# Three small weight computations of an attention stage: from VectorE to GpSimd

## The reference

```python
B, H, S, D = 4, 8, 576, 64
a = softmax(causal(q @ k.T / sqrt(D)));  local = a @ v
q_p = phi(q)                      # phi(x) = x + 1 for x > 0, else exp(x)
mem_out = (q_p @ M_prev) / (q_p @ z_prev + 1e-6)
g = sigmoid(beta)                 # one gate for each head
attn = g * mem_out + (1 - g) * local
# then x = attn as (2304, 512); two layers up/down, 512 -> 2048 -> 512,
# the first with a clipped square as activation, the second with silu
```

## Time and profile before

| | us |
|---|---|
| median of 3 runs | 987.01 (986.19 to 989.4) |
| the profiled execution | 988.2 |
| its span in the trace | 986.1 |
| attention stage: until TensorE's first feed-forward matmul | 193.6 |

### The profile page before, as it was taken

One profiled execution on the slowest core, in us unless ns is written; L12 is line 12 of the kernel. 1 busy time (PEld: TensorE's weight loads), 2 busy tenths in 40 slices (PEclk: granted clock), 3 DMA queues, 4 the chain that ended last, 5 costly groups with the idle time before them and its releaser, 6 DMA issues.

```text
span 986.1 us, 14130 instructions
## 1 busy us (share of the span) xinstructions
PE 975.1 (99%) x5468; PEld 816.0 (83%) x5468; DVE 474.3 (48%) x946; ACT 384.1 (39%) x847; POOL 285.6 (29%) x304
## 2 busy tenths in 40 slices
PE   7999999999999999999999999999999999999998
PEld 6888877888888888888888998888888888888897
DVE  6999999756344434434434663323332332322232
ACT  6988888633223222322223332322222232222232
POOL 6989999799000000000000798000000000000000
PEclk8999999999999999999999999999999999999999
DMA  6555544244000000000000343001000100100010
GB/s 196 150 157 154 168 145 131 71 119 117 22 1 1 1 0 1 1 1 1 1 1 1 86 129 97 0 1 43 1 1 1 44 0 1 43 1 1 1 44 22
DMA packets 38401, 48.10 MB, mean 49 GB/s; under 512 B 3264, under 2 KB 21696, under 8 KB 38336
## 3 DMA queue, kind: packets, MB, share of 16 engines
q1 hardware_dynamic: 38336, 47.20, 15.9%
HBM read 42.47 MB, written 4.72 MB: 48 GB/s over the span
## 4 chain that ended last, share of the span: by engine, by line
PE 83%; DVE 8%; POOL 3%; issue 2%; ACT 2%; DMA 1%; SPq 0%; POOLq 0%; DVEq 0%
PE ps L1021 26%; PE ps L1023 26%; PE ps L1022 26%; PE ps L899 2%; PE ps L954 1%; DVE prob L653 1%; DVE qlo L635 1%; PE ps L862 1%; DVE ptail L653 1%; DVE mden L659 1%; DVE rw L685 1%; POOL phir L358 1%; ACT prob L476 1%; DVE glo L797 1%; POOL phs L386 1%
## 5 line engine op out<-in xcount | busy, mean ns | idle before, releaser
L1021 PE MATMUL ps<-xhi,W 128*128 128x512 f32 (+1 forms) x640 | 235.4, 368 | 0.0
L1022 PE MATMUL ps<-xlo,W 128*128 128x512 f32 (+1 forms) x640 | 235.4, 368 | 0.0
L1023 PE MATMUL ps<-xhi,W 128*128 128x512 f32 (+1 forms) x640 | 235.4, 368 | 0.0
L797 DVE TENSOR_TENSOR glo<-act_t,ghi 128x512 fp32r<-128x512 f32 (+1 forms) x160 | 118.0, 738 | 223.6 <-ACT ghi L576 223.6
L576 ACT CAST ghi<-act_t 128x512 fp32r<-128x512 f32 (+1 forms) x160 | 92.5, 578 | 235.4 <-PE ps L1023 213.1
L1021 PEld LDWEIGHTS ps<-xhi,W 128*128 128x128 f32 x640 | 120.7, 189 | 20.7
L1022 PEld LDWEIGHTS ps<-xlo,W 128*128 128x128 f32 x640 | 120.6, 188 | 20.4
L1023 PEld LDWEIGHTS ps<-xhi,W 128*128 128x128 f32 x640 | 120.6, 188 | 20.2
L335 POOL CAST W<-stage 128x512 fp32r<-128x512 f32 x64 | 46.2, 722 | 303.0 <-PE ps L1023 300.6
L568 ACT ACTIVATE act_t<-act_t,half_col 128x512 f32<-128x512 f32 (+1 forms) x80 | 54.5, 681 | 185.7 <-DVE act_t L790 185.7
L1021 PE MATMUL ps<-ghi,W 128*128 128x512 f32 (+1 forms) x320 | 118.1, 369 | 0.3 <-DVE glo L797 0.2
(11 more groups left out here) (113 smaller groups left out, 1336.5 us busy)
## 6 DMA issues: line engine op xcount, KB each, us to landing
stage<-in_moe_w_in SPq DMA_DIRECT2D x32, 256.0 KB, 2.7
stage<-in_moe_w_out SPq DMA_DIRECT2D x32, 256.0 KB, 2.7
vn<-in_vN SPq DMA_DIRECT2D x16, 320.0 KB, 5.0
qraw<-in_qT SPq DMA_DIRECT2D x15, 320.0 KB, 3.2
qn<-in_qN SPq DMA_DIRECT2D x16, 288.0 KB, 4.9
zb<-in_zN SPq DMA_DIRECT2D x32, 144.0 KB, 3.6
out_x<-ostage SPq DMA_DIRECT2D x17, 256.0 KB, 2.0
kraw<-in_kT SPq DMA_DIRECT2D x15, 288.0 KB, 2.9
```

Of the source, the lines that this page charges most:

```text
L797: nc.vector.tensor_tensor(glo[:, f % SLOTS, 0:TN[tile]], a, ghi[:, f % SLOTS, 0:TN[tile]].bitcast(F32), ALU.subtract).then_inc(glo_done, 1)
L1021: nc.tensor.matmul(dst, w_lo_, x_hi_, start=first, stop=False)
L1022: nc.tensor.matmul(dst, w_hi_, x_lo_, start=False, stop=False)
L1023: return nc.tensor.matmul(dst, w_hi_, x_hi_, start=False, stop=last)
```

## The change

GpSimd computes three things that VectorE computed: the gate's product (into a new tile `share`), phi's weights `rw[:, 1]`, and the last block's weights `rwt`. GpSimd does them between `phi_sum_1(p+1)` and `weigh(p)`, each waiting for the one before it. VectorE keeps the reduce, the addition of 1e-9 and the two reciprocals. In the first pair VectorE does `rows` ahead of `norms`.

```diff
+        share = sb("share", [P, NB], where=att)
+            def shares(p):
+                pool.wait_ge(norm_step, 2 * p + 2)
+                if p == 0:
+                    pool.wait_ge(gate_step, 5)
+                nc.gpsimd.tensor_tensor(share[:], mden[:, 1], gcols[:, p % PAIRS, :], ALU.mult).then_inc(gated, 1)
+
+            def weights(p):
+                pool.wait_ge(gated, p + 1)
+                pool.wait_ge(row_step, 2 * p + 1)
+                nc.gpsimd.tensor_tensor(rw[:, 1, :], den[:], share[:], ALU.mult).then_inc(row_made, 1)
+                pool.wait_ge(row_step, 2 * p + 2)
+                pool.wait_ge(row_made, 2 * p + 1)
+                nc.gpsimd.tensor_tensor(rwt[:], rw[:, :, 2 * FULL:].broadcast_to([P, 2, 2]),
+                                        bd[:].unsqueeze(1).broadcast_to([P, 2, 2]), ALU.mult).then_inc(row_made, 1)
+
             def weigh(p):
-                pool.wait_ge(row_step, 4 * p + 4)
+                pool.wait_ge(row_made, 2 * p + 2)
...
             for p in range(NPAIR):
                 if 0 < p < NPAIR - 1:
                     phi_sum_1(p + 1)
+                shares(p)
+                weights(p)
                 weigh(p)
                 widen(p)
...
-                elif step == 1:
-                    dve.wait_ge(norm_step, 3 * p + 1)
+                else:
+                    dve.wait_ge(norm_step, 2 * p + 1)
                     if p:
-                        dve.wait_ge(row_step, 4 * p - 1)
+                        dve.wait_ge(gated, p)
                     nc.vector.reciprocal(mden[:, 1], mden[:, 0]).then_inc(norm_step, 1)
-                else:
-                    dve.wait_ge(norm_step, 3 * p + 2)
-                    dve.wait_ge(gate_step, 5)
-                    nc.vector.tensor_tensor(mden[:, 1], mden[:, 1], gcols[:, p % PAIRS, :],
-                                            ALU.mult).then_inc(norm_step, 1)
...
                 if step == 0:
                     dve.wait_ge(exp_done, NB * p + NB)
+                    if p:
+                        dve.wait_ge(row_made, 2 * p)
                     nc.vector.tensor_scalar(den[:], rowsum[:, p % 2, :], 1e-9, None, ALU.add).then_inc(row_step, 1)
...
-                elif step == 2:
-                    dve.wait_ge(norm_step, 3 * p + 3)
-                    if p:
-                        dve.wait_ge(weighed, 2 * p)
-                    nc.vector.tensor_tensor(rw[:, 1, :], den[:], mden[:, 1], ALU.mult).then_inc(row_step, 1)
-                else:
-                    nc.vector.tensor_tensor(rwt[:], rw[:, :, 2 * FULL:].broadcast_to([P, 2, 2]),
-                                            bd[:].unsqueeze(1).broadcast_to([P, 2, 2]), ALU.mult).then_inc(row_step, 1)
...
                 if p == 0:
+                    for step in range(2):
+                        rows(0, step)
                     norms(0, 0)
                     norms(0, 1)
-                    norms(0, 2)
-                    for step in range(4):
-                        rows(0, step)
```

More of the change, by code:

```diff
@@ L189, in build @@
         norm_step, row_step, row_wide = sem("norm_step"), sem("row_step"), sem("row_wide")
+        gated, row_made = sem("gated"), sem("row_made")
         weighed, v_done = sem("weighed"), sem("v_done")
@@ L464, in phi_part_2 @@
                 if p >= 2:
-                    act.wait_ge(norm_step, 3 * p - 5)
+                    act.wait_ge(norm_step, 2 * p - 3)
                 nc.scalar.activation(phie[p % 2][:, :, 0:D], phir[p % 3][:], ACT.Exp, scale=-1.0).then_inc(phi_part, 1)
@@ L673, in rows @@
                     dve.wait_ge(exp_done, NB * p + NB)
+                    if p:
+                        dve.wait_ge(row_made, 2 * p)
                     nc.vector.tensor_scalar(den[:], rowsum[:, p % 2, :], 1e-9, None, ALU.add).then_inc(row_step, 1)
-                    return
-                dve.wait_ge(row_step, 4 * p + step)
-                if step == 1:
+                else:
+                    dve.wait_ge(row_step, 2 * p + 1)
                     if p:
@@ L775, in _ @@
                 if more:
-                    for step in range(3):
+                    for step in range(2):
                         norms(p + 1, step)
```

## The result

The changed kernel takes 989.12 us (median of 22 runs, 987.8 to 990.88), the one before 986.86 (22 runs, 985.93 to 989.4). The ratio is 1.0024, with a 95% interval of 1.0018 to 1.0030: slower by 2.3 us, inside the 0.3% that I took for no change, and clear of zero. Predicted were +0.8 us and the range 984.3 to 992.0.

The account below looks back on a forecast made before the run. Attention pairs were bound by TensorE and GpSimd; GpSimd's added chain, 15 x 0.80, less 11.3 us of former waits, gave +0.7, so 988.9 profiled and 987.8 us as median, range 984.3 to 992.0.

Parts of the forecast that it names:

- TensorE's floor: Attention stage: TensorE needs 11.05 us a pair without a split; the stage holds 3.1 + 0.5 = 3.6 us above that.
- GpSimd becomes the sole bound of pairs 5 to 14: Two pairs would take GpSimd 23.16 us, before 22.70, against 22.10 for TensorE.
- c: GpSimd's three added dependent operations, from the end of L353 to the start of L386: 0.80 us, bounded by 0.40 and 1.15.
- the line through L389 and L386: GpSimd tensor_tensor length from two rows: 1.67 ns an element and 0.19 fixed, hence 0.20 to 0.21 for small ones.
- 15c - 11.3: Shift of the kernel's end: 15 times c, minus GpSimd's former waits for VectorE; here +0.7 us.
- L386 of pairs 2, 8, 14 and 15: Forecast start times of GpSimd's `weigh` in these pairs: near 41.4, 109.1, 178.5 and 187.5 us.
- The wait of 2.54 in the last pair: GpSimd's former wait for VectorE in pair 15; it would absorb most of the delay, from +2.6 to +0.9 us.
- TensorE's scores are late by 0.65: GpSimd's `high_k(15)` in pair 13 comes 2.1 us later, VectorE wins back 1.47, so scores are 0.65 late.
- by way of L377: Last pair: L377, which TensorE's L933 needs, comes 0.9 us later, so L933 and all after it 0.7 later.
- VectorE wins 1.47 at a turn with a hold: Turn like pair 8's: VectorE's L664 to L711 shrinks from 1.92 to 0.45 us, so L711 comes 1.47 earlier.
- case 4: Rival: L674 or L680 on VectorE would still be held by GpSimd, end about +2 us; chance 0.02.
- The collisions of L627 and L635 with GpSimd's large operations: Assumption for every pair: these VectorE instructions' collisions with GpSimd keep the same sum; L627 stays at about 1.24 us.

Follow-up runs that it names:

- psum_all: Kernel before, all small work still on VectorE, with the gated norm and the last block's two factors in an idle PSUM bank: 983.3 us, ratio 0.9964.
- after_nov: Changed kernel without GpSimd's product of the values with 1 - g: 982.9 us, 0.9960 of the kernel before.
- before_nov: Kernel before without GpSimd's product of the values with 1 - g: 982.4 us, ratio 0.9961.
- one_more: Changed kernel with the gate's product made twice, one more 128 x 9 operation in GpSimd's chain: 992.6 us, 1.0060 of the kernel before.
- psum_ptr: psum_all with rwt made by two tensor_scalar, tensor from PSUM and per-partition scalar from SBUF: 985.7 us, 0.9997 of the kernel before.

## Why the prediction was right, point by point

- *TensorE's floor, 3.6 us below the kernel before.* Right: by their ratios psum_all, after_nov and before_nov lie 3.6, 3.9 and 3.8 below, and 3.6 is inside the interval of each. (124.73 less 121.55 is 3.2 and not 3.1, so the sum of the rows is 3.7.)
- *GpSimd becomes the sole bound of pairs 5 to 14, and pays c in each pair.* Right, and shown: 97% busy, 12.6 and 10.7 for the two kinds of pairs (predicted 12.53 and 10.63), and one_more moved the end by 3.5 to 3.9 us for one more operation in each pair.
- *c = 0.80.* Mis-sized: 0.88. The three spans are 0.20, 0.21 and 0.20, as the line through L389 and L386 gave. Two of the three gaps are 0.08. The third, ahead of L396, is 0.15 in every pair. I don't know why that one is longer; L396 waits for two semaphores, but so does L393.
- *The end moves by 15c - 11.3.* With 0.88 that is +1.9. The spans give +1.7, the stage +2.1, the medians +2.3. The predicted +0.7 was too small by 15 x 0.08 = 1.2 us of c, and by the 0.2 of room that it saw between the end of L377 and the start of L933 in the last pair. Little of that was room: in the changed kernel L939 still starts 0.14 behind the end of L379, and the end moved by as much as L379 did.
- *L386 of pairs 2, 8, 14 and 15 near 41.4, 109.1, 178.5 and 187.5.* L403 came at 41.22, 109.30, 179.28 and 188.26. The fixed point of the forecast, L353 in pair 1 at 28.62, is at 28.20 here (L355), because this execution began earlier by 0.42. Counted from it, the four are 0.24, 0.62, 1.20 and 1.18 later than forecast, close to n x 0.08, as an error in c must be.
- *The wait of 2.54 in the last pair swallows most of the delay.* Right: L403 is 3.4 late in pair 14 and 1.7 in pair 15.
- *TensorE's scores are late by 0.65, and the end, by way of L377, by 0.7.* Right in kind: two ways, almost equal, L377's a little longer. They came at 1.43 and 1.69. With 13 x 0.08 more in c, 0.15 less won by VectorE and the start 0.42 earlier, the 0.65 becomes 1.42.
- *VectorE wins 1.47 at a turn with a hold.* Nearly: 1.32. L683 to L718 takes 0.60, not 0.45, because L690 takes 0.30 and not 0.16.
- *"L674 and L680 run at 0.16 and 0.22 under the same L353"; case 4 has a chance of 0.02.* This step is wrong, though it cost little. L674 started at 105.92 and L353 at 105.93: it was under way when GpSimd began, and the row shows nothing of a hold. `tensor_scalar` with its one tensor in SBUF is held. The changed kernel has it once at full length (L355 runs from 71.04 to 72.45, and L690, in VectorE's timeline, until 72.48), and for a rest of 0.14 at most turns:

```profile
71.13 1.35 DVE L690 TENSOR_SCALAR den<-rowsum 128x9 f32<-128x9 f32 x1 [0.24 <-ACT ptail L495]
72.52 0.21 DVE L695 RECIPROCAL rw<-den 128x9 f32<-128x9 f32 x1
```

So the change leaves one of VectorE's small instructions open to the hold, and the general sentence, that an instruction with a single SBUF operand isn't held, is wrong. For L680 the reading was right: it ran short in the middle of L353.
- *The collisions of L627 and L635 with GpSimd's large operations stay what they were.* Right in the sum: at the turn to pair 8 L365, L373 and L355 take 1.92, 1.83 and 1.42, 5.2 together, and their three counterparts before took 1.94, 1.84 and 1.42. L646 takes 1.24 as L627 did. At the turn to pair 7 the parts did change: 1.93, 1.84 and 1.42 where it was 1.43, 1.78 and 2.00, and L646 takes 1.24 where L627 took 1.55. But these three are 5.2 together both times.

The mechanism was the one forecast, a full GpSimd that pays for each pair. The size was off by a factor of nearly three, most of it in c, a term that is multiplied by 15.

## What to carry to other kernels

When an engine that has no idle time left takes over even 0.2 us in each turn of a loop, the price is nearly that time, plus its gap to the next dependent instruction, times the turns; what the other engine wins turns up as its wait for the first. Look at who is full before asking who is held: in this kernel the hold went away by itself when GpSimd had slack. To free a VectorE product of two SBUF tiles from GpSimd, one operand can be put in an idle PSUM bank: in psum_all that gave 3.6 us with nothing added to GpSimd. It isn't free of cost, for TensorE must wait for the bank, and psum_ptr, without a hold in its `rwt`, gave 0.3. And before reading "ran short beside it" from two rows, compare their starts.

## What the runs showed of the hardware

- A VectorE instruction can be held by GpSimd with one SBUF tensor as well. Held, which means that the row lasts until that of GpSimd's instruction ends: `tensor_tensor` with two SBUF tensors (1.02), `tensor_scalar` from SBUF to SBUF with a constant (128 x 9: 1.35 and 0.74, unheld 0.16) and with a per-partition scalar (128 x 2 and 128 x 3: 1.09 and 1.08 for two, unheld 0.49). Not held: `reciprocal` (0.21), `tensor_tensor` with one tensor in PSUM (0.14 to 0.17), `tensor_scalar` with its tensor in PSUM and its scalar in SBUF (0.22 at most).
- The holds of `tensor_scalar` fit a rule of the Trainium skill, VectorE: DVE Perf Modes, "What auto-detection actually checks": an instruction with one source runs on both ports when source and destination are in SBUF and their outer counts are both even or equal. With SBUF — State Buffer, "Who interferes with whom", which names `copy`, `cast` and `tensor_scalar` as the ones that can contend in that way, it covers the widths 9, 3 and 2. The `reciprocal`, 9 to 9 in SBUF, isn't among those named, and wasn't held (0.21). The trace shows the holds; that this mode is their cause is an inference.
- GpSimd's `tensor_tensor` of 4 to 9 elements takes 0.20 to 0.22, and the next dependent instruction starts 0.08 later, in one place 0.15.
